# Joins and norm sums moved in an attention recurrence, and the routing to experts begun and ordered anew

## The reference

```python
# B, H, S, D = 4, 8, 768, 48
mag = np.sqrt(a_re * a_re + a_im * a_im)
scale = np.minimum(mag, 0.999) / (mag + 1e-06)
a_re_n, a_im_n = (a_re * scale, a_im * scale)
for t in range(S):
    new_re = ar * S_re - ai * S_im          # ar, ai: a_re_n, a_im_n of step t
    new_im = ar * S_im + ai * S_re
    S_re, S_im = (new_re + k_t v_t^T, new_im)
    y[:, :, t] = q_t @ S_re
# x: 3072 tokens x 384
x = np.maximum(np.maximum(x @ w1, x @ w2), x @ w3) @ w_out     # d_ff 768
xn = x / (np.linalg.norm(x, axis=-1, keepdims=True) + 1e-06)
logits = xn @ en.T / tau                                       # 8 experts
expert_idx = np.argmax(logits, axis=1); probs = softmax(logits)
for e in range(8):
    mask = expert_idx == e
    h = np.maximum(x[mask] @ w1[e], 0.0)                       # 384 -> 1024 -> 384
    out[mask] = gate_w[mask, None] * (h @ w2[e])
```

## Time and profile before

| | before |
|---|---|
| median of 3 runs | 990.97 us (989.76 to 991.07) |
| profiled execution | 990.71 us, of which its span 989.0 |
| TensorE busy | 873.7 us (88%) |
| VectorE busy | 656.4 us (66%) |
| GpSimd busy | 491.1 us (50%) |
| ACT busy | 461.2 us (47%) |
| mean granted TensorE clock | 0.943 of full speed |

### The profile page before, as it was taken

The page is one execution under the profiler, slowest core; times in us unless marked ns, Lnnn a source line. Parts: engine busy times, 40 slices in busy tenths (PEclk is TensorE's granted clock), DMA queues, the critical chain, the costliest instruction groups (busy, mean ns, idle before and its releaser), DMA issues.

```text
span 989.0 us, 18419 instructions
## 1 busy us (share of the span) xinstructions
PE 873.7 (88%) x6398; PEld 776.1 (78%) x6399; DVE 656.4 (66%) x1054; ACT 461.2 (47%) x859; POOL 491.1 (50%) x888
## 2 busy tenths in 40 slices
PE   0568887999989999999999999839999999999995
PEld 0445777888878898889889888838888888888785
DVE  5968677898799989999876755267323252556721
ACT  5765635555555566565344442233222242446521
POOL 1290998199998989889791000023222222223221
PEclk9767889999989999999999999967999999999998
DMA  9204232542414243331321110334411151416311
GB/s 302 65 20 106 73 81 68 139 106 71 118 53 112 87 118 87 93 86 54 87 64 40 38 46 19 139 137 167 168 40 40 40 168 40 167 34 210 121 40 32
DMA packets 42247, 90.80 MB, mean 92 GB/s; under 512 B 6312, under 2 KB 23728, under 8 KB 40768
## 3 DMA queue, kind: packets, MB, share of 16 engines
q1 hardware_dynamic: 38080, 77.48, 26.1%
q0 software_dynamic: 4096, 12.40, 4.0%
HBM read 70.20 MB, written 18.48 MB: 90 GB/s over the span
## 4 chain that ended last, share of the span: by engine, by line
PE 52%; DVE 17%; POOL 11%; ACT 6%; issue 5%; DMA 5%; SPq 2%; DVEq 0%; ACTq 0%; POOLq 0%
PE mm L1570 6%; PE mm L1574 5%; PE mm L1571 5%; PE yu L1570 4%; PE tr L1570 4%; PE tr L1571 4%; PE tr L1574 4%; PE yu L1571 4%; PE yu L1574 4%; POOL c_im L1889 3%; PE mm L1808 3%; POOL c_re L1888 3%; POOL ring L1891 2%; POOL ring L1892 2%; PE sc L1627 2%
## 5 line engine op out<-in xcount | busy, mean ns | idle before, releaser
L1570 PE MATMUL mm<-up_hi,x_hi 128*128 128x384 f32 x432 | 160.0, 370 | 34.2 <-DVE h_sb L1109 12.1
L1888 POOL TENSOR_TENSOR c_re<-ring 112x128 f32<-112x128 f32 x165 | 102.4, 620 | 108.0 <-DMA ring<-an_scratch 60.1
L1571 PE MATMUL mm<-up_lo,x_hi 128*128 128x384 f32 x432 | 149.9, 347 | 0.0
L1966 POOL DMA_INDIRECT out_rows<-g_o,rows_out x30 | 34.7, 1155 | 182.0 <-DVE g_o L1487 182.0
L1570 PEld LDWEIGHTS mm<-up_hi,x_hi 128*128 128x128 f32 x432 | 83.5, 193 | 50.6 <-DVE h_sb L1109 15.5
L952 ACT ACTIVATE g_h<-tr 128x512 f32<-128x512 f32 x60 | 35.8, 597 | 171.6 <-PE tr L1574 166.1
L1889 POOL TENSOR_TENSOR c_im<-ring 112x128 f32<-112x128 f32 x165 | 109.3, 662 | 0.0
L1574 PE MATMUL mm<-up_hi,x_lo 128*128 128x384 f32 x432 | 101.8, 345 | 0.0
L1891 POOL TENSOR_TENSOR ring<-c_re,c_im 112x64 f32<-112x64 f32 x165 | 83.8, 508 | 12.9
L1892 POOL TENSOR_TENSOR ring<-c_re,c_im 112x64 f32<-112x64 f32 x165 | 86.8, 526 | 0.0
L1109 DVE TENSOR_TENSOR h_sb<-mm,h_sb 128x384 f32<-128x384 f32 x96 | 52.9, 551 | 48.5 <-PE mm L1574 46.4
(11 more groups left out here) (242 smaller groups left out, 2093.2 us busy)
## 6 DMA issues: line engine op xcount, KB each, us to landing
raw<-in_moe_w SPq DMA_DIRECT2D x16, 1536.0 KB
a_dn<-in_a_laid SPq DMA_DIRECT2D x20, 384.0 KB, 7.2
an_scratch<-a_dn SPq DMA_DIRECT2D x20, 384.0 KB, 2.3
ring<-an_scratch SPq DMA_DIRECT2D x20, 384.0 KB, 6.2
q_in<-in_q_laid SPq DMA_DIRECT2D x24, 224.0 KB, 3.0
k_in<-in_k_laid SPq DMA_DIRECT2D x24, 224.0 KB, 3.2
v_in<-in_v_laid SPq DMA_DIRECT2D x24, 192.0 KB, 3.3
x_scratch<-x_sb SPq DMA_DIRECT2D x24, 192.0 KB, 2.7
```

The lines of the kernel that those rows point to most:

```text
L1570: nc.tensor.matmul(out, hi[:, x, :], w_hi(x), start=(x == 0), stop=False)
L1571: nc.tensor.matmul(out, hi[:, x, :], w_lo(x), start=False, stop=False)
L1888: nc.gpsimd.tensor_tensor(c_re[:, 0:count, :, :], cur, bc(prev[:, :, 0, :], 2, 2), ALU.mult).then_inc(chain_prod, 1)
```

## The change

1. `norms_in`: unit 10 is done in pass 4 with unit 11, not in pass 3 with unit 9.
2. Joins: group 2's, all in pass 2 before, stand as one late in pass 2 and two early in pass 3, where `late_z` now holds too. Group 5's first join goes from late in pass 7 to early in pass 8.
3. Ahead of the loop and in passes 0 and 1, the steps of units 4 and 5 go forward between joins and z steps, and in pass 1 the joins stand ahead of `rotation` and the second unit's `norm_m2`.
4. `norm_sum` of each pass stands ahead of `z_newton`, not behind the third `moe_max`.
5. Routing: VectorE and ACT begin without waiting for the stores of x (`x2_stored`); only GpSimd, which gathers from them, waits. ACT splits two parts of expert 0 ahead of the gates' exponential. VectorE computes the places and all one-hot matrices ahead of the gates. The gate products go from GpSimd to VectorE, behind `fetch`. TensorE's 24 gate products go behind the up products of the first expert tile, and VectorE's tables into that tile.

```diff
-            first = 6 if n == 1 else n + 6 if n < 4 else n + 7
-            count = 2 if n in (1, 3) else 1
+            first = 6 if n == 1 else n + 6 if n < 5 else n + 7
+            count = 2 if n in (1, 4) else 1
...
-        for g in range(DIRECT, NG):
-            joins_early[2 * g - 2] = [(g, 0), (g, 1)] if g < 5 else [(g, 1)]
+        joins_late[2] = [(2, 0)]
+        joins_early[3] = [(2, 1), (2, 2)]
+        for g in range(3, NG):
+            joins_early[2 * g - 2] = [(g, 0), (g, 1)] if g < 6 else [(g, 1)]
             joins_late[2 * g - 2] = [(g, 2)]
-            if g >= 5:
+            if g >= 6:
                 joins_late[2 * g - 3] = [(g, 0)]
...
+            norm_square(5, norm_of(5))
+            norm_mag(4, norm_of(4))
             stage_z(0)
             z_square(0)
-            norm_square(5, norm_of(5))
+            norm_mag(5, norm_of(5))
             z_recip(0)
-            norm_mag(4, norm_of(4))
-            norm_mag(5, norm_of(5))
...
-                late_z = n == 1
+                late_z = n in (1, 3)
...
-            for number in range(7):
+            for number in range(4):
                 join(0, number)
             norm_m2(4, norm_of(4))
+            for number in range(4, 7):
+                join(0, number)
+            norm_m2(5, norm_of(5))
+            norm_sum(4, norm_of(4))
             z_norm(0)
-            norm_m2(5, norm_of(5))
+            norm_sum(5, norm_of(5))
             z_newton(0)
...
                 if now:
                     add_state(n)
+                for m in norms:
+                    norm_sum(m, norm_of(m))
                 if more:
                     z_newton(n + 1)
                 if prev:
                     moe_max(n - 1, 0, 2)
-                for m in norms:
-                    norm_sum(m, norm_of(m))
...
             dve.wait_ge(x2_taken, 2 * NC)
-            dve.wait_ge(x2_stored, 16 * NC)
...
+            for x in range(2):
+                nc.vector.tensor_tensor(gate_hot[:, :, x, :], in_slot[:, :, :], bc(gate_parts[:, x, :].bitcast(F32), 2, SLOTS), ALU.mult) \
+                    .then_inc(gates_hot, 1)
             for n in range(KX):
                 split_lo(0, n)
...
+            def expert_tile(t, split=None, very_first=False):
+                if very_first:
+                    tables()
                 gx_move(t + 1)
...
+                if very_first:
+                    gates()
                 wait(pe, ght_ready, 2 * t)
...
-            pool.wait_ge(in_slots, 1)
-            for x in range(2):
-                nc.gpsimd.tensor_tensor(gate_hot[:, :, x, :], in_slot[:, :, :], bc(gate_parts[:, x, :].bitcast(F32), 2, SLOTS), ALU.mult) \
-                    .then_inc(gates_hot, 1)
             pool.wait_ge(x2_stored, 16 * NC)
```

## The result

The changed kernel has a median of 996.56 us in 5 runs (995.50 to 999.71), the kernel before 990.43 beside it (988.37 to 991.07). The ratio is 1.0075, its 95% interval 1.0060 to 1.0090, so +7.4 us, with some 1.5 on either side; the two medians alone are 6.1 apart. 990.7 was forecast, with a range up to 996.5 and 0.29 for slower. The profiled execution took 999.71, the slowest of the five together with one other: its +9.0 in the span contains about 2 to 3 us that most executions don't have.

A forecast was written before the change was run, and what follows sets the result against it. No engine was taken as the bound throughout, so each edit was priced in its own stretch. The terms 0.5 − 13.6 + 11.0 − 0.5 − 6.6 + 2.8 + 6.3 + 0 gave −0.1, so 990.7 us, range 983 to 996.5.

The forecast's parts named there:

- The sum ahead of `z_newton`: Even passes 6 to 16: z_newton waits for norm_sum, which waits for ACT; six times 1.05, +6.3 us.
- D: Rival: TensorE's holes in passes 8 and 10 grow until the clock falls, +1.5 each, 993.7 us; chance 0.09.
- −0.5: Pass 4: it starts from a quieter VectorE, −0.5 us.
- The 0 for the odd passes: Odd passes: moving norm_sum costs 0, because VectorE waits for the chain later anyway.
- Group 2: Pass 2: the wait for the chain and pass 3's two-unit norm work go, interval 35.4 becomes 21.8, −13.6 us.
- Passes 3 to 4: Moved joins and two-unit norm pass bring holes and slow clock, +11.0 us; then pass 4 −0.5.
- Pass 7: The stall of 5.14 at VectorE's join of group 5 goes, 28.4 becomes 21.8, −6.6 us.
- the join's price in pass 8: Group 5's join now stands in front of z_norm in pass 8 and delays h_sb, +2.8 us, between 0 and 5.2.
- Prologue: Ahead of the loop: first scores 2.3 later, nearly all recovered in passes 0 and 1; +0.5 us, between 0 and 2.3.
- Routing: Between attention and experts: first up product 4.2 earlier, taken back by gate products and tile 1's wait; sum 0, −4.2 to +3.
- Rival C: Expert 0's first tile: the clock falls and down products take twice 4.24 us, 994.9 us; chance 0.14.
- the rule cited there: Routing: two-SBUF-input VectorE work contends with GpSimd's SBUF reads; its row copy could wait, sum up to 1.0 us higher.

The follow-up runs named there:

- e6_no_sum: The changed kernel with norm_sum put back behind the third moe_max in every pass; 983.91 us, ratio 0.9952 to the kernel before.
- e13_sum_even: The kernel before with norm_sum ahead of z_newton only in the even passes from 4 on; 998.06 us, ratio 1.0081.
- e7_no_prologue: The changed kernel with the code ahead of the loop and passes 0 and 1 as before; 994.50 us, ratio 1.0064 to the kernel before.
- e8_groups: The kernel before with only the joins of groups 2 and 5 and unit 10 moved as in the change; 987.06 us, ratio 0.9987.
- e2_group2: The kernel before with only unit 10 moved to pass 4 and group 2's joins and late_z as changed; 985.17 us, ratio 0.9950.
- 12: The changed kernel with norm_sum back behind the third moe_max and group 5's first join back in pass 7; 983.58 us, ratio 0.9927 to the kernel before.
- 15: The changed kernel with group 5's join as before and norm_sum directly behind z_newton; 980.58 us, ratio 0.9917 to the kernel before.
- e5_prologue: The kernel before with only the moves of units 4 and 5 ahead of the loop and in passes 0 and 1; 989.69 us, ratio 0.9998.
- e14_sum_odd: The kernel before with norm_sum ahead of z_newton only in the odd passes from 5 on; 988.72 us, ratio 0.9991.

## Why the prediction was wrong, step by step

**The sum ahead of `z_newton`: right mechanism, half the size.** This is the term that failed: +6.3 forecast, +7.3 measured alone, about +12 in the changed kernel. Everything else together was forecast at −6.4 and measured at −4.8 (`e6_no_sum`). With the 7.3 that the sum costs alone in its place, the forecast would have been +0.9 for the +7.4 measured. What is missing is the 5 by which the sum costs more among the other moves: the terms were added as if none depended on another. Three things in the term itself were off.
First, the price in a pass. I took 1.05, 1.54 on `z_newton` less 0.46 given back. From the mark to the product behind `x_hi` it was 15.82 in pass 10 before (328.45 to 344.27) and is 17.29 now (330.82 to 348.11): 1.5. TensorE's waits for that product in the even passes from 6 to 14 went from at most 1.0 to between 1.4 and 2.2.
Second, the clock. With a hole of 2.1 the granted clock falls in some passes (the 0.66 at 348.11), which I had only as a rival, D, at 0.09. Pass 10 became 3.0 longer, 1.5 of it the wait, the rest behind the fall.
Third, the count. I counted six passes and left out pass 4, which has two sums and two early joins; its interval grew by 3.8 where I had −0.5. In `e13_sum_even` it grew by 1.7 with nothing else changed. Pass 8, which I counted, hardly belongs in the changed kernel: it took 25.04 without the sum (`e6_no_sum`) and 25.13 with it.
The 0 for the odd passes was right, but not for the reason given. VectorE waits for the chain in pass 7 and in no other odd pass. What differs is ACT: in the changed kernel `norm_sum` waits 1.49 or 1.50 for `norm_mag` in passes 4, 6, 8, 10, 14 and 16 (0.78 in 12), and not at all in the odd passes from 5 on.

**Why alone 7.3 and together 12.** This stays open; the traces show one piece. With the sum moved alone, pass 7 begins 2.05 later and ends 3.9 earlier. VectorE reaches the join of group 5 at 268.77 for 266.03 and the chain releases it at 269.80 for 271.17, so it waits 1.03 for 5.14. TensorE's hole is 0.86 for 4.28, and the mean granted clock of the pass 1.00 for 0.88: 28.44 becomes 22.52, 5.9 given back, 3.4 of it by the hole and 2.5 by the products that ran at half clock behind it. In the changed kernel the moves of the joins have taken that stall away already, and the moved sum gives nothing back there. But this can't be the whole: in `e7_no_prologue` and `e8_groups` pass 7 has no stall either (21.61 in both), and yet the one is only 7.6 above the other, with the sum and the routing (0.9 alone) between them, no more than the sum costs alone. The price of 12 was measured only with the prologue there, and no run has the sum and the prologue without the rest. The intervals of such differences are 2 to 3 wide on either side.

**Group 2 (−13.6, measured −7.6 from mark to mark, −10.0 for the end of pass 2).** The step "Pass 2 loses the wait for the chain" took the chain's end, 133.14, as given. It depends on what VectorE does meanwhile: the chain took 37.87 for 33.85. Five other kernels with this move (2, 6, 7, 12 and 15 above) release the join between 136.36 and 136.64, and in 6, 7, 12 and 15 it waits 2.67 to 5.12 for that and TensorE idles 3.2 to 4.4 behind it. In `e8_groups` VectorE comes later and waits for nothing. Pass 2 still ends 13.4 to 15.8 earlier than before, as much as was forecast, since the rest of the work has left it. In the profiled execution of the changed kernel the chain also started 2.8 later, which `e5_prologue` and `e6_no_sum`, with the same prologue, don't show (100.18 and 98.68), and that is where the missing 3 us are. Group 2 alone came to −5.0, where my terms said −3.1.
**Passes 3 to 4 (+11.0, measured +9.3)** is right with its parts: holes of 1.45 and 2.79 behind `h_sb` for the 2.2 and 2.9 forecast, a half-clock product behind the second, and the two-unit pass's hole of 2.63 for 3.38. Without the sum (`e6_no_sum`) passes 3 and 4 together took 59.32 for 48.26, +11.1 where +10.5 was forecast.
**Pass 7 (−6.6, measured −6.8)** is right in size; and the join's price in pass 8 (+2.8) too: `e6_no_sum` and `e8_groups`, without the sum, have 25.04 and 24.80 there for 21.78.
**Prologue (+0.5):** nothing measured alone, within its bounds; the replay it came from is in no row.
**Routing (0):** +0.9 us by the ratio, −0.4 to +2.2; `row_hot` 0.90 for the 0.95 assumed, `fetch` 4.6 earlier for 4.2, gate products 2.76 for 2.65, the wait for tile 1's rows 1.33 for 1.5. Rival C, the clock falling behind the gate products, did not come: the first down product, at 692.58, takes 0.42. Nor did the gather become the last: `rows_in` took 1.05 beside the gate product. It had taken 1.04 before, beside a split (`e_lo`) that reads two SBUF inputs as well, and takes 0.18 later, beside neither; so the rule cited there holds for it, but the price was in the time before already.
**The tail.** 1.9 us were lost behind 634.68, where TensorE's wait for `x_hi` (1.95 for 1.62) is followed by a half-clock stretch (granted 0.68 from 635 to 640). The same interval is 21.19 in the profile of the kernel before, but 22.77 in that of `e2_group2`, 22.89 in `e5_prologue` and 23.00 in `e14_sum_odd`, so it belongs to the spread of single executions and not to the change.

## What to carry to other kernels

Before an instruction is moved ahead on a queue, ask which engine feeds it and how long that feed lies behind the one of the instruction that it overtakes: a 0.5 us sum cost 1.5 us a pass because ACT did its input second, and two instructions further back it cost nothing. Don't add the terms of moves that meet in the same waits: here the single ones added to +1.1 and the change cost 7.4. A stall on a slow chain can hide a delay of the passes in front of it, so try such moves together as well as alone. And work moved in front of such a wait isn't free if it shares SBUF reads with the engine that is waited for.

## What the runs showed of the hardware

VectorE's work from two SBUF inputs stretches GpSimd's work from SBUF: 3.1 us more for a chain of 60 short instructions when 4.5 us were added beside it, 0.15 for the same time with one input. A GpSimd product of 112x128 takes 0.46 alone or beside a VectorE instruction with one input in PSUM, 0.79 and 0.91 beside one with two in SBUF.

The same hole of TensorE did not always bring the clock down. In the kernel before and in `e8_groups` the same product waits the same 1.95 us, in the same place of pass 6; the windows of a microsecond some 5 us behind the hole's end (granted clock is the third number from the end) show full clock in the one and 0.50 in the other, where it had fallen before: 0.64 is the mean from 241.1 to 246. TensorE did the same products before and behind the hole in both. I have no explanation that these traces show.

```profile
244.87 0.45 PE L1570 MATMUL mm<-up_hi,x_hi 128*128 128x384 f32 x1 [1.95 <-ACT h_sb L735]
```

```profile
250.00:251.00 1.00, 0.87 (x5) 0.90 (x6) 1.00 (x4) 1.00 (x2) 0.92 (x3) 1.00 1.01 354
```

```profile
241.11 0.44 PE L1572 MATMUL mm<-up_hi,x_hi 128*128 128x384 f32 x1 [1.95 <-ACT h_sb L737]
```

```profile
246.00:247.00 1.00, 1.00 (x9) 0.94 (x10) 1.00 (x2) 1.00 (x3) 0.92 (x4) 0.50 0.99 353
```
